# Three pairs of score banks, and row maxima as single-bank units, in a fused attention and mixture-of-experts kernel

## The chip, the cores and the metric

The kernel runs on one core of a Trainium2 chip. The time is device microseconds (us) of one execution, the median of several runs. The engines that matter here are TensorE (PE, with its weight loads as PEld), VectorE (DVE), ScalarE (ACT) and GpSimd (POOL); SyncE (SP) issues nearly all transfers. They run side by side and meet only at semaphores.

## The reference

The change lies in the first of three stages, attention over 32 heads (4 batches by 8), 1152 keys of 64 numbers, and 576 queries after pooling by two:

```python
q_pool = q.reshape(B, H, S // factor, factor, D).mean(axis=3)
scores = scale * np.matmul(q_pool, k.transpose(0, 1, 3, 2))
scores = scores - np.max(scores, axis=-1, keepdims=True)
attn = np.exp(scores)
attn = attn / (np.sum(attn, axis=-1, keepdims=True) + 1e-09)
return np.matmul(attn, v).astype(np.float32)
```

Two mixture-of-experts stages follow (from about 440 us on); the change doesn't touch them.

## The kernel before, in words

PSUM has eight banks of 512 fp32 per partition, and `ps` is all of them. The head size is 64, half of the array's 128 rows, so the operands lie twice: even and odd tiles of keys and of queries are on partitions 0 to 63 (half 0, `rows_of(0)`) and 64 to 127 (half 1, `rows_of(1)`). Matmuls of the two halves go to different banks.

**Scores.** A head n has nine steps, `scores(n, s)`. A step is eight matmuls, four parts (L652, L654, L656, L658: high by high, low by high, high by low, and the row maximum with its sign turned) on each half, each 288 columns wide, accumulated into a pair of banks, one bank for a half. ScalarE then takes the exponential of the pair into `probs` (`exp_step`, L1067). The pair alternates between banks 0/1 and 2/3 (`step_bank`), and a step waits until the exponential of the step two before it is done.

**Row maxima.** The maximum over the keys must be known before a head's scores are made, so it is found one head ahead: while head n's scores are made, `row_max(n + 1, j)` makes single-pass scores of head n+1, and VectorE reduces them (`top_of_rows`). There are six jobs to a head. Five are a matmul of 512 keys on each half (L620) into a pair of banks, reduced by one instruction of 2x512 (L1357); the one with j=4 is five small matmuls for the last 128 keys (L613, L615) and two reductions (L1351, L1353). The jobs alternate between bank pairs 6/7 and 4/5 and stand before the steps s = 0, 2, 3, 4, 6, 7 (`JOB_STEPS`). A job waits until the job two before it is reduced. `join_tops` (L1364) joins the maxima into `neg_max`.

**End of a head.** TensorE's queue then has `turn(n+2, 0)` and `turn(n+2, 1)` (transposes of the keys and queries of head n+2, L580 to L591, into banks 6 and 7 and a tail bank), `turn_neg_max(n+1)` (L629, a transpose that waits for `join_tops(n+1)`), `weigh(n)` (36 matmuls of the probabilities with the values into bank 4, L675) and `add_up(n)` (the sums, L686). ScalarE meanwhile rounds the turned operands (`round_k`, `round_q`), places the maxima (`place_neg_max`) and reads the result out of bank 4 (`read_x`). VectorE makes the low parts (`low_k`, `low_q`, `low_ends`) and adds one pair of probabilities (`add_pair`, L1384). GpSimd adds the other probabilities (L498 to L512) and divides.

Each engine's order is written out by hand: the loop at the end of the TensorE block, and the like for the others. TensorE works strictly in that order, so what stands behind a waiting instruction waits too.

Of the kernel before, what the change touches and what calls it, by code (L numbers as in the profile page):

```python
# [8 lines left out]
ALU = mybir.AluOpType  # L9
ACT = mybir.ActivationFunctionType  # L10
AX = mybir.AxisListType
P = 128
# [4 lines left out]
def soft_moe_chain(nc, q, k, v, phi, w1, w2, w_in, w_out, out):  # L17
# [47 lines left out]
    JOBS = QT + 1  # L65
    KP = (NT - 1) // 2 * P
# [102 lines left out]
    with ExitStack() as ctx:  # L169
# [39 lines left out]
        def job_bank(m, j):  # L209
            if m == 0:  # L210
                return 2 if j % 2 == 0 else 4
            return 6 if j % 2 == 0 else 4

        def step_bank(n, s):
            if n == HEADS - 1:
                return (2, 0, 6)[s % 3]
            return 2 * ((n + s) % 2)

        def tail_bank(m):
            if m < 2:  # L220
                return 1 - m
            return 2 * ((m + 1) % 2) + 1
# [4 lines left out]
        def turned_q(odd):  # L227
            return ps[rows_of(odd), 7, 0:QF // 2 * P].rearrange("r (a c) -> r a c", c=P)
# [339 lines left out]
        def _(pe):  # L568
            JOB_STEPS = (0, 2, 3, 4, 6, 7)

            def turn(m, j):

                if m == 1:
                    pe.wait_ge(max_free, 1)
                elif m > 1:
                    pe.wait_ge(max_free, JOBS * m - 1)
                if j == 0:
                    pe.wait_ge(k_loaded, 32 * m + 32)
                    for t in range(NT // 2):
                        mm = pe.transpose(ps[:, 6, P * t:P * t + P],  # L580
                                          k_raw[:, 2 * t:2 * t + 2, :].rearrange("p t d -> p (t d)"), ident[:])
                else:
                    pe.wait_ge(q_pooled, m + 1)
                    for t in range(QF // 2):
                        pe.transpose(ps[:, 7, P * t:P * t + P], q_pool[:, 2 * t:2 * t + 2, :].rearrange("p two d -> p (two d)"),  # L585
                                     ident[:])
                    if m >= 2:
                        pe.wait_ge(exp_done, NT * (m - 2) + NT - 1)
                    pe.transpose(ps[:, tail_bank(m), 0:P], k_raw[:, NT - 1:NT + 1, :].rearrange("p two d -> p (two d)"),
                                 ident[:])  # L590
                    mm = pe.transpose(ps[:, tail_bank(m), P:2 * P],  # L591
                                      q_pool[:, QF:QT + 1, :].rearrange("p two d -> p (two d)"), ident[:])
                mm.then_inc(turned, 1)

            def row_max(m, j):

                if m == 0 and j in (0, QF):
                    pe.wait_ge(rounded, 5 if j == 0 else ROUNDS)
                if j == 0:
                    if m > 0:  # L600
                        pe.wait_ge(turn_free, 2 * m + 2)
                elif j == 1:
                    if m > 1:
                        pe.wait_ge(x_read, m - 1)
                    if m > 0:
                        pe.wait_ge(max_free, JOBS * m)
                else:
                    pe.wait_ge(max_free, JOBS * m + (j - 1))
                if j == QF:
                    b = job_bank(m, j)  # L610
                    for t in (0, 2, 1, 3):
                        g = t // 2
                        pe.matmul(ps[:, b + g, P * (t % 2):P * (t % 2) + P], q_hi[m % 2][rows_of(g), P * t:P * t + P],  # L613
                                  k_hi[m % 2][rows_of(g), KP:KP + P], start=True, stop=True)
                    mm = pe.matmul(ps[:, b, 2 * P:3 * P], q_hi[m % 2][rows_of(0), P * QF:P * QT],  # L615
                                   k_hi[m % 2][rows_of(0), KP:KP + P], start=True, stop=True)
                else:
                    t = min(j, QF)
                    for g in range(2):
                        mm = pe.matmul(ps[:, job_bank(m, j) + g, :], q_hi[m % 2][rows_of(g), P * t:P * t + P],  # L620
                                       k_hi[m % 2][rows_of(g), 0:KP], start=True, stop=True)
# [9 lines left out]
            def scores(n, s):  # L631

                if s == 0:
                    pe.wait_ge(neg_free, n + 1)
                    if n > 0:
                        pe.wait_ge(turn_free, 2 * min(n + 2, HEADS))
                if n == 0 and s == 0:
                    pe.wait_ge(turn_free, 3)
                if n == HEADS - 1 and s >= 2:
                    pe.wait_ge(exp_done, NT * n + max(s - 2, 0))  # L640
                elif NT * n + s >= 2:
                    pe.wait_ge(exp_done, NT * n + s - 1)
                b0 = step_bank(n, s)
                for part in range(4):
                    for g in range(2):
# [15 lines left out]
            def weigh(n):  # L661
# [6 lines left out]
                if n + 1 < HEADS:  # L668
                    pe.wait_ge(max_free, JOBS * (n + 1) + JOBS)
# [59 lines left out]
            row_max(0, 0)  # L729
            row_max(0, 1)  # L730
            warm(5, 0)
            row_max(0, 2)
            turn(1, 0)
            row_max(0, 3)
            turn(1, 1)
            row_max(0, 4)
            row_max(0, 5)
# [313 lines left out]
        def _(act):  # L1051
# [31 lines left out]
            def round_k(m):  # L1083
                act.wait_ge(turned, 2 * m + 1)
                high(k_hi[m % 2][:, 0:KP], ps[:, 6, :])

            def round_q(m):
                kh, qh, b = k_hi[m % 2], q_hi[m % 2], tail_bank(m)
                act.wait_ge(turned, 2 * m + 2)
                for g in range(2):  # L1090
                    for odd in range(2):
                        high(by_turns(qh, g, odd), turned_q(odd))
                high(kh[:, KP:KP + P], ps[:, b, 0:P])
                high(qh[:, P * QF:SQ], ps[:, b, P:P + QLAST])
# [206 lines left out]
        def _(dve):  # L1301
# [29 lines left out]
            def low_k(m):  # L1331
                dve.wait_ge(rounded, ROUNDS * m + 1)
                low(k_lo[m % 2][:, 0:KP], ps[:, 6, :], k_hi[m % 2][:, 0:KP]).then_inc(turn_free, 1)

            def low_q(m):
                dve.wait_ge(rounded, ROUNDS * m + 5)
                for g in range(2):
                    for odd in range(2):
                        low(by_turns(q_lo[m % 2], g, odd), turned_q(odd), by_turns(q_hi[m % 2], g, odd))

            def low_ends(m):
                b = tail_bank(m)
                dve.wait_ge(rounded, ROUNDS * m + ROUNDS)
                low(k_lo[m % 2][:, KP:KP + P], ps[:, b, 0:P], k_hi[m % 2][:, KP:KP + P])
                low(q_lo[m % 2][:, P * QF:SQ], ps[:, b, P:P + QLAST], q_hi[m % 2][:, P * QF:SQ]).then_inc(turn_free, 1)

            def top_of_rows(m, j):
                dve.wait_ge(max_full, JOBS * m + j + 1)
                if j == QF:
                    b = job_bank(m, j)  # L1350
# [3 lines left out]
                else:  # L1354
                    t, b = min(j, QF), job_bank(m, j)
# [3 lines left out]

            def join_tops(m):  # L1360
                dve.wait_ge(max_free, JOBS * m + JOBS)
# [37 lines left out]

            def tops(m, invert):  # L1400
                for j in range(JOBS):
                    top_of_rows(m, j)
                    if j == 3 and invert:
# [5 lines left out]
            tops(0, False)  # L1409
# [224 lines left out]
```

## Time and profile before

| | |
|---|---|
| median of 3 runs (lowest to highest) | 740.65 us (740.49 to 741.43) |
| the profiled execution | 741.45 us, of which its span is 739.7 us |
| TensorE / VectorE / ScalarE / GpSimd busy over the span | 98% / 71% / 62% / 65% |
| heads | 32, one about every 13.5 us, to about 440 us |
| granted TensorE clock, mean | 0.993 |

Busy times are sums of instruction durations, and matmuls overlap: a TensorE that is shown busy may still stand between two streams. A matmul's duration includes its way through the array, so the pace is read from the distance between two starts, not from the durations. The chain of work that ended last follows, from the end backwards, what released each instruction. Times of day in the rows below are in microseconds from the start of the span.

### The profile page before, as it was taken

The numbers are of one execution on the slowest core, as the hardware profiler recorded it, in microseconds if no ns is written. First come the engines' busy times: TensorE is split into PE (matmuls) and PEld (weight loads), VectorE is DVE, ScalarE is ACT, GpSimd is POOL, SyncE is SP. The second block draws the span as 40 slices with busy tenths as digits, with TensorE's granted clock in tenths as the row PEclk, the third lists the DMA queues.
The fourth block names the chain that finished last, engine by engine and source line by source line (L and its number), as shares of the span: only waits on it lengthen the run. The fifth ranks groups of instructions, "written<-read, shape, count | busy, mean of one in ns | idle before, by whom it ended". The sixth has DMA issues, their size and how long they took to land.

```text
span 739.7 us, 17095 instructions
## 1 busy us (share of the span) xinstructions
PE 726.1 (98%) x6375; PEld 541.8 (73%) x6375; DVE 524.3 (71%) x828; ACT 455.1 (62%) x1008; POOL 483.7 (65%) x429
## 2 busy tenths in 40 slices
PE   6999999999999999999999999999999999999997
PEld 5777777777777767777777677434778888888886
DVE  7888888888888888888888847533895555455542
ACT  4677776776777767767767763214665454545453
POOL 1588888888888888888888872212774444444442
PEclk9899999999999999999999999999999999999999
DMA  5123435334334353343443347899301010101011
GB/s 147 41 59 84 122 92 156 103 106 155 88 104 159 90 156 104 98 164 88 124 139 88 96 140 263 299 386 375 138 0 43 1 43 0 43 0 43 0 43 43
DMA packets 51623, 81.83 MB, mean 111 GB/s; under 512 B 14556, under 2 KB 20572, under 8 KB 51548
## 3 DMA queue, kind: packets, MB, share of 16 engines
q1 hardware_dynamic: 51180, 80.37, 34.8%
q8 instruction: 48, 0.79, 0.4%
q10 hardware_dynamic: 368, 0.46, 0.2%
q14 instruction: 27, 0.22, 0.1%
HBM read 75.94 MB, written 4.79 MB: 109 GB/s over the span
## 4 chain that ended last, share of the span: by engine, by line
PE 94%; DVE 3%; issue 1%; POOL 1%; ACT 1%; POOLq 0%; DVEq 0%; ACTq 0%
PE ps L675 20%; PE ps L652 9%; PE ps L982 8%; PE ps L981 8%; PE ps L980 8%; PE ps L620 6%; PE ps L654 5%; PE ps L656 5%; PE ps L658 5%; PE ps L686 3%; PE ps L580 3%; PE ps L970 2%; PE ps L864 2%; PE ps L894 2%; PE ps L585 1%
## 5 line engine op out<-in xcount | busy, mean ns | idle before, releaser
L1067 ACT ACTIVATE probs<-ps 128x576 f32<-128x576 f32 x288 | 183.7, 651 | 45.1 <-PE ps L658 31.4
L1357 DVE TENSOR_REDUCE mx<-ps 128x2 f32<-128x1024 f32 (+1 forms) x160 | 189.4, 1218 | 29.9 <-PE ps L620 27.9
L546 POOL TENSOR_TENSOR g_lo<-g_buf,g_hi 128x384 fp32r<-128x384 f32 x96 | 102.1, 1065 | 100.9 <-ACT g_hi L1242 100.9
L675 PE MATMUL ps<-probs,v_sb 128*64 128x288 f32 x1152 | 146.8, 409 | 0.1
L509 POOL TENSOR_TENSOR p_sum<-p_sum,probs 128x576 f32<-128x576 f32 x93 | 129.1, 1415 | 0.0
L1585 DVE SCALAR_TENSOR_TENSOR v_buf<-u_buf 128x384 f32<-128x384 f32 x96 | 60.4, 629 | 86.4 <-ACT u_buf L1235 85.8
L675 PEld LDWEIGHTS ps<-probs,v_sb 128*64 128x64 f32 x1152 | 79.6, 137 | 56.4 <-issue 5.2
L1235 ACT ACTIVATE u_buf<-ps,half 128x384 f32<-128x384 f32 x96 | 55.7, 581 | 93.9 <-PE ps L970 93.9
L980 PE MATMUL ps<-wo_hi,g_hi 128*128 128x512 f32 x282 | 110.4, 391 | 0.6 <-POOL g_lo L546 0.5
L982 PE MATMUL ps<-wo_lo,g_hi 128*128 128x512 f32 x282 | 110.8, 393 | 0.0
L981 PE MATMUL ps<-wo_hi,g_lo 128*128 128x512 f32 x282 | 110.6, 392 | 0.0
L652 PE MATMUL ps<-q_hi,k_hi 64*128 64x288 f32 x576 | 102.0, 337 | 0.7 <-ACT q_neg L1100 0.7
L654 PE MATMUL ps<-q_hi,k_lo 64*128 64x288 f32 x576 | 88.6, 293 | 0.0
L656 PE MATMUL ps<-q_lo,k_hi 64*128 64x288 f32 x576 | 88.6, 293 | 0.0
L658 PE MATMUL ps<-q_neg,k_one 64*128 64x288 f32 x576 | 88.2, 291 | 0.0
L498 POOL TENSOR_TENSOR p_sum<-probs 128x576 f32<-128x576 f32 x32 | 45.6, 1425 | 50.3 <-ACT probs L1067 50.3
L620 PE MATMUL ps<-k_hi,q_hi 64*128 64x512 f32 x320 | 70.5, 427 | 3.2 <-DVE mx L1357 2.1
L652 PEld LDWEIGHTS ps<-q_hi,k_hi 64*128 64x128 f32 x576 | 56.0, 186 | 23.9 <-ACT probs L1067 21.7
L980 PEld LDWEIGHTS ps<-wo_hi,g_hi 128*128 128x128 f32 x282 | 53.0, 188 | 14.3 <-issue 2.7
L1329 DVE TENSOR_TENSOR q_lo<-ps,q_hi 64x256 fp32r<-64x256 f32 (+1 forms) x160 | 60.5, 379 | 2.5 <-ACT q_hi L1081 1.2
L982 PEld LDWEIGHTS ps<-wo_lo,g_hi 128*128 128x128 f32 x282 | 53.0, 188 | 11.4
L654 PEld LDWEIGHTS ps<-q_hi,k_lo 64*128 64x128 f32 x576 | 58.1, 187 | 2.7
(216 smaller groups left out, 1252.1 us busy)
## 6 DMA issues: line engine op xcount, KB each, us to landing
pre<-in_moe_w SPq DMA_DIRECT2D x41, 512.0 KB, 4.9
v_sb<-in_v SPq DMA_DIRECT2D x32, 288.0 KB, 2.9
k_raw<-in_k SPq DMA_DIRECT2D x31, 288.0 KB, 3.8
q_raw<-in_q SPq DMA_DIRECT2D x32, 256.0 KB, 4.0
from_x<-in_moe_w SPq DMA_DIRECT2D x9, 512.0 KB, 5.1
p_inv<-inv_dram SPq DMA_DIRECT2D x62, 72.0 KB, 2.7
out<-o_stage SPq DMA_DIRECT2D x34, 128.0 KB, 2.3
staged<-in_moe_w SPq DMA_DIRECT2D x8, 512.0 KB, 5.5
```

Source lines behind the costliest of these rows:

```text
L509: nc.gpsimd.tensor_tensor(total, total, probs[:, u, :], ALU.add).then_inc(probs_added, 1)
L620: mm = pe.matmul(ps[:, job_bank(m, j) + g, :], q_hi[m % 2][rows_of(g), P * t:P * t + P], k_hi[m % 2][rows_of(g), 0:KP], start=True, stop=True)
L652: mm = pe.matmul(out, k_hi[n % 2][rows, t], q_hi[n % 2][rows, cols], start=True, stop=False)
L654: mm = pe.matmul(out, k_lo[n % 2][rows, t], q_hi[n % 2][rows, cols], start=False, stop=False)
L656: mm = pe.matmul(out, k_hi[n % 2][rows, t], q_lo[n % 2][rows, cols], start=False, stop=False)
L658: mm = pe.matmul(out, k_one[rows, :], q_neg[n % 2][rows, cols], start=False, stop=True)
L675: mm = pe.matmul(ps[D * h:D * h + D, 4, 0:HALF], v_sb[n % 2][:, u, :], probs[:, u, HALF * h:HALF * h + HALF], start=(i == 0), stop=(i == N ...
L980: pe.matmul(o, g_hi[par][:, f, toks], wo_hi[:, f, :], start=(f == 0), stop=False)
L981: pe.matmul(o, g_lo[par][:, f, toks], wo_hi[:, f, :], start=False, stop=False)
L982: mm = pe.matmul(o, g_hi[par][:, f, toks], wo_lo[:, f, :], start=False, stop=(f == NF - 1))
L1067: nc.scalar.activation(dst, ps[:, b0:b0 + 2, 0:HALF], ACT.Exp, scale=SCORE_SCALE).then_inc(exp_done, 1)
L1357: top = nc.vector.tensor_reduce(mx[0:w, NC * t:NC * t + 2], ps[0:w, b:b + 2, :], AX.X, ALU.max)
```

## The change

- Scores use three pairs of banks in turn: 2(n mod 2), the other of 0/1 and 2/3, and 4/5. The wait of a step is now for the exponential of the step three before it. Steps 1 and 2 of a head wait for the turned operands of head n+2 to be split and for `read_x` instead.
- From head 1 on, the maxima are made in 12 single-bank units (`UNITS`) in place of 6 jobs in pairs: ten of one matmul of 512 keys on one half, then three and two small matmuls. Unit u uses half u mod 2 and bank 6 + u mod 2, and from u = 2 on waits until unit u-2 is reduced. Unit s stands before step s, and units 9, 10 and 11 stand behind the last step. Head 0 keeps the six jobs.
- VectorE reduces each unit by an instruction of its own, with one more for the last 64 queries: 13 for a head where there were 7.
- In heads 1 to 30, even steps begin with half 1.
- The turned operands and the maxima use the banks of the scores; the turns wait for exponentials, not for reductions.
- `weigh` no longer waits for the reductions, and `low_q` waits for all of ScalarE's roundings.

```diff
+    UNITS = 2 * QF + 4
...
-        def job_bank(m, j):
-            if m == 0:
-                return 2 if j % 2 == 0 else 4
-            return 6 if j % 2 == 0 else 4
+        def job_bank(j):
+            return 2 if j % 2 == 0 else 4
+
+        def unit_bank(u):
+            return 6 + u % 2
...
         def step_bank(n, s):
-            if n == HEADS - 1:
-                return (2, 0, 6)[s % 3]
-            return 2 * ((n + s) % 2)
-
-        def tail_bank(m):
+            if s % 3 == 2:
+                return 6 if n == HEADS - 1 else 4
+            return 2 * ((n + s % 3) % 2)
+
+        def keys_bank(m):
+            return 6 if m < 2 else 2 * (m % 2)
+
+        def queries_bank(m):
+            return 7 if m < 2 else 2 * (m % 2) + 1
...
-                if m == 1:
-                    pe.wait_ge(max_free, 1)
-                elif m > 1:
-                    pe.wait_ge(max_free, JOBS * m - 1)
+                if m >= 2:
+                    pe.wait_ge(exp_done, NT * (m - 2) + NT - 2)
...
+            def row_max(m, u):
+
+                if u == 0:
+                    pe.wait_ge(turn_free, 2 * m + 2)
+                if u >= 2:
+                    pe.wait_ge(max_free, units_of(m) + (u - 1))
+                b, g = unit_bank(u), u % 2
+                if u < UNITS - 2:
+                    t = u // 2
+                    mm = pe.matmul(ps[:, b, :], q_hi[m % 2][rows_of(g), P * t:P * t + P], k_hi[m % 2][rows_of(g), 0:KP],
+                                   start=True, stop=True)
+                else:
+                    tiles = (0, 1, QF) if g == 0 else (2, 3)
+                    for i, t in enumerate(tiles):
+                        mm = pe.matmul(ps[:, b, P * i:P * i + P], q_hi[m % 2][rows_of(g), P * t:P * t + P],
+                                       k_hi[m % 2][rows_of(g), KP:KP + P], start=True, stop=True)
                 mm.then_inc(max_full, 1)
...
-                if n == HEADS - 1 and s >= 2:
-                    pe.wait_ge(exp_done, NT * n + max(s - 2, 0))
-                elif NT * n + s >= 2:
-                    pe.wait_ge(exp_done, NT * n + s - 1)
+                    if n == 0:
+                        pe.wait_ge(turn_free, 3)
+                if s == 1 and 0 < n < HEADS - 1:
+                    pe.wait_ge(turn_free, 2 * n + 4)
+                if s == 2 and 0 < n < HEADS - 1:
+                    pe.wait_ge(x_read, n)
+                if s >= 3:
+                    pe.wait_ge(exp_done, NT * n + s - 2)
...
-                if n + 1 < HEADS:
-                    pe.wait_ge(max_free, JOBS * (n + 1) + JOBS)
...
                 for s in range(NT):
-                    if n + 1 < HEADS and s in JOB_STEPS and (n > 0 or s > 0):
-                        row_max(n + 1, JOB_STEPS.index(s))
-                    scores(n, s)
+                    if n + 1 < HEADS and (n > 0 or s > 0):
+                        row_max(n + 1, s)
+                    scores(n, s, (1, 0) if s % 2 == 0 and 0 < n < HEADS - 1 else (0, 1))
...
+                if n + 1 < HEADS:
+                    for u in range(NT, UNITS):
+                        row_max(n + 1, u)
                 if n + 2 < HEADS:
                     turn(n + 2, 0)
```

TensorE in the middle of head 1, before: a job's two matmuls (both halves), then a step, whose first matmul waits for an exponential.

```order
L620 MATMUL ps<-k_hi_62,q_hi_66 128x512 [waits max_free]
L620 MATMUL ps<-k_hi_62,q_hi_66 128x512
L652 MATMUL ps<-q_hi_67,k_hi_63 128x288 [waits exp_done]
L652 MATMUL ps<-q_hi_67,k_hi_63 128x288
L654 MATMUL ps<-q_hi_67,k_lo_65 128x288 x2
L656 MATMUL ps<-q_lo_71,k_hi_63 128x288 x2
L658 MATMUL ps<-q_neg_69,k_one 128x288 x2
```

The same place after the change (lines are those of the changed kernel): one matmul of one half stands before each step.

```order
L632 MATMUL ps<-k_hi_62,q_hi_66 128x512 [waits max_free]
L669 MATMUL ps<-q_hi_67,k_hi_63 128x288 [waits exp_done]
L669 MATMUL ps<-q_hi_67,k_hi_63 128x288
L671 MATMUL ps<-q_hi_67,k_lo_65 128x288 x2
L673 MATMUL ps<-q_lo_71,k_hi_63 128x288 x2
L675 MATMUL ps<-q_neg_69,k_one 128x288 x2
L632 MATMUL ps<-k_hi_62,q_hi_66 128x512 [waits max_free]
```

The matmul of 512 was a pair before five of the nine steps, and is now a single one before each of them.

TensorE at the end of head 1, before: the last step is followed by the turns at once.

```order
L658 MATMUL ps<-q_neg_69,k_one 128x288 x2
L580 MATMUL ps<-ident,k_raw 128x128 [waits k_loaded,max_free]
L580 MATMUL ps<-ident,k_raw 128x128 x3
L585 MATMUL ps<-ident,q_pool 128x128 [waits q_pooled,max_free]
L585 MATMUL ps<-ident,q_pool 128x128
L589 MATMUL ps<-ident,k_raw 128x128 [waits exp_done]
L591 MATMUL ps<-ident,q_pool 128x128
```

After the change:

```order
L675 MATMUL ps<-q_neg_69,k_one 128x288 x2
L632 MATMUL ps<-k_hi_62,q_hi_66 128x512 [waits max_free]
L637 MATMUL ps<-k_hi_62,q_hi_66 128x128 [waits max_free]
L637 MATMUL ps<-k_hi_62,q_hi_66 128x128 x2
L637 MATMUL ps<-k_hi_62,q_hi_66 128x128 [waits max_free]
L637 MATMUL ps<-k_hi_62,q_hi_66 128x128
L589 MATMUL ps<-ident,k_raw 128x128 [waits k_loaded,exp_done]
L589 MATMUL ps<-ident,k_raw 128x128 x3
L596 MATMUL ps<-ident,q_pool 128x128 [waits q_pooled,exp_done]
```

Units 9, 10 and 11 now stand between the last step and the turns, each with a wait for VectorE.

VectorE's maxima of one head, before, and then after:

```order
L1357 TENSOR_REDUCE mx<-ps 128x2 [waits max_full] x4
L1370 RECIPROCAL p_spread<-p_spread 64x9 [waits sums_spread]
L1351 TENSOR_REDUCE mx<-ps 128x4 [waits max_full]
L1353 TENSOR_REDUCE mx<-ps 64x1
L1357 TENSOR_REDUCE mx<-ps 64x2 [waits max_full]
L1364 TENSOR_REDUCE neg_max<-mx 128x2x5 [waits neg_full,max_free]
```

```order
L1383 TENSOR_REDUCE mx<-ps 128x1 [waits max_full] x8
L1403 RECIPROCAL p_spread<-p_spread 64x9 [waits sums_spread]
L1383 TENSOR_REDUCE mx<-ps 64x1 [waits max_full] x2
L1385 TENSOR_REDUCE mx<-ps 128x2 [waits max_full]
L1389 TENSOR_REDUCE mx<-ps 64x1
L1385 TENSOR_REDUCE mx<-ps 128x2 [waits max_full]
L1397 TENSOR_REDUCE neg_max<-mx 128x2x5 [waits neg_full,max_free]
```

Seven reductions and the joining one became thirteen and the joining one; the reciprocal of the sums keeps its place after two thirds of the wide ones.

## Rows read from the trace of the kernel before

**Rows 1.** The page: chain of waits, shares of the span by engine and line

```profile
PE 94%; DVE 3%; issue 1%; POOL 1%; ACT 1%; POOLq 0%; DVEq 0%; ACTq 0%
```

**Rows 2.** One head in four stretches: busy us (instructions) of PE, PEld, DVE, ACT, POOL; clock

```profile
209.62:216.82 7.20, 7.20 (x92) 6.21 (x88) 6.59 (x8) 5.79 (x10) 5.56 (x6) 1.00 0.19 47
216.82:217.95 1.13, 1.13 (x12) 0.96 (x10) 0.30 (x2) 1.02 (x2) 1.13 (x2) 1.00 0.01 0
217.95:222.46 4.51, 4.51 (x37) 2.49 (x36) 3.98 (x7) 3.21 (x12) 4.26 (x4) 1.00 0.38 120
222.46:223.09 0.63, 0.63 (x18) 0.40 (x16) 0.31 (x2) 0.00 (x0) 0.55 (x2) 1.00 0.98 387
```

**Rows 3.** Timeline of TensorE in that head: start, us (of the group), line, operands, count

```profile
209.62 0.50 PE L620 MATMUL ps<-k_hi,q_hi 64*128 64x512 f32 x2
209.96 0.30 PE L652 MATMUL ps<-q_hi,k_hi 64*128 64x288 f32 x2
...
210.49 0.30 PE L652 MATMUL ps<-q_hi,k_hi 64*128 64x288 f32 x2
...
211.01 0.40 PE L620 MATMUL ps<-k_hi,q_hi 64*128 64x512 f32 x2
211.40 0.40 PE L652 MATMUL ps<-q_hi,k_hi 64*128 64x288 f32 x2
...
214.50 0.27 PE L615 MATMUL ps<-k_hi,q_hi 64*128 64x128 f32 x1
214.52 0.43 PE L652 MATMUL ps<-q_hi,k_hi 64*128 64x288 f32 x2
...
215.15 0.43 PE L620 MATMUL ps<-k_hi,q_hi 64*128 64x512 f32 x2
215.38 0.33 PE L652 MATMUL ps<-q_hi,k_hi 64*128 64x288 f32 x2
```

**Rows 4.** Timeline of the weight loads, same head, with idle time before and its releaser

```profile
211.40 0.19 PEld L652 LDWEIGHTS ps<-q_hi,k_hi 64*128 64x128 f32 x2 [0.32 <-ACT probs L1067]
211.51 0.19 PEld L654 LDWEIGHTS ps<-q_hi,k_lo 64*128 64x128 f32 x2
...
216.81 0.42 PEld L580 LDWEIGHTS ps<-ident,k_raw 128*128 128x128 f32 x4 [0.16 <-issue]
...
217.64 0.14 PEld L629 LDWEIGHTS ps<-ident,neg_max 128*128 128x128 f32 x1
217.95 0.20 PEld L675 LDWEIGHTS ps<-probs,v_sb 128*64 128x64 f32 x4 [0.17 <-issue]
```

**Rows 5.** Waits from 20 to 440 us: total us, times, longest

```profile
PEld ps L652 <- ACT probs L1067: 21.7, 92, 0.3
```

**Rows 6.** Timeline of ScalarE: two exponentials

```profile
210.69 1.20 ACT L1067 ACTIVATE probs<-ps 128x576 f32<-128x576 f32 x2 [0.17 <-PE ps L658]
```

**Rows 7.** Timeline of VectorE, same head

```profile
212.60 2.35 DVE L1357 TENSOR_REDUCE mx<-ps 128x2 f32<-128x1024 f32 x2
...
214.86 0.20 DVE L1370 RECIPROCAL p_spread<-p_spread 64x9 f32<-64x9 f32 x1
214.98 0.62 DVE L1351 TENSOR_REDUCE mx<-ps 128x4 f32<-128x512 f32 x1
215.52 0.28 DVE L1353 TENSOR_REDUCE mx<-ps 64x1 f32<-64x128 f32 x1
215.72 1.21 DVE L1357 TENSOR_REDUCE mx<-ps 64x2 f32<-64x1024 f32 x1
216.97 0.19 DVE L1364 TENSOR_REDUCE neg_max<-mx 128x10 f32<-128x30 f32 x1
218.14 0.69 DVE L1329 TENSOR_TENSOR k_lo<-ps,k_hi 128x512 fp32r<-128x512 f32 x1 [0.99 <-ACT k_hi L1081]
```

**Rows 8.** Timeline of GpSimd: its last sum of the head

```profile
220.15 1.80 POOL L512 TENSOR_TENSOR p_sum<-p_sum,p_sum 128x576 f32<-128x576 f32 x1
```

More of the change, by code:

```diff
@@ L583, in turn @@
                     pe.wait_ge(q_pooled, m + 1)
+                    if m == 1:
+                        pe.wait_ge(max_free, 1)
                     for t in range(QF // 2):
[L585 to L590, printed above, removed]
@@ L593, in turn, with row_max_first @@
                 mm.then_inc(turned, 1)
-            def row_max(m, j):
-                if m == 0 and j in (0, QF):
+            def row_max_first(j):
+                if j in (0, QF):
                     pe.wait_ge(rounded, 5 if j == 0 else ROUNDS)
[L599 to L608, printed above, removed]
+                if j > 1:
+                    pe.wait_ge(max_free, j - 1)
+                b = job_bank(j)
@@ L609, in row_max @@
                 if j == QF:
-                    b = job_bank(m, j)
                     for t in (0, 2, 1, 3):
                         g = t // 2
[L613 to L616, printed above, removed]
+                        pe.matmul(ps[:, b + g, P * (t % 2):P * (t % 2) + P], q_hi[0][rows_of(g), P * t:P * t + P],
+                                  k_hi[0][rows_of(g), KP:KP + P], start=True, stop=True)
@@ L617, in row_max @@
+                    mm = pe.matmul(ps[:, b, 2 * P:3 * P], q_hi[0][rows_of(0), P * QF:P * QT],
+                                   k_hi[0][rows_of(0), KP:KP + P], start=True, stop=True)
                 else:
@@ L629, in turn_neg_max, with scores @@
                 pe.transpose(ps[:, neg_bank(m), 0:P], neg_max[:, :], ident[:]).then_inc(neg_full, 1)
-            def scores(n, s):
+            def scores(n, s, halves):
                 if s == 0:
                     pe.wait_ge(neg_free, n + 1)
[L635 to L638, printed above, removed]
-                if n == HEADS - 1 and s >= 2:
-                    pe.wait_ge(exp_done, NT * n + max(s - 2, 0))
-                elif NT * n + s >= 2:
-                    pe.wait_ge(exp_done, NT * n + s - 1)
+                    if n == 0:
[6 more added lines that the diff above has]
+                    pe.wait_ge(exp_done, NT * n + s - 2)
                 b0 = step_bank(n, s)
                 for part in range(4):
-                    for g in range(2):
+                    for g in halves:
                         rows = rows_of(g)
@@ L1354, in top_of_rows @@
                 else:
-                    t, b = min(j, QF), job_bank(m, j)
+                    t = min(j, QF)
                     w = q_cols(t)[1]
@@ L1398, in top_logits, with tops_first @@
                                         negate=True).then_inc(l_neg_ready, 1)
+            def tops_first():
+                for j in range(JOBS):
+                    top_of_rows_first(j)
+                join_tops(0)
             def tops(m, invert):
-                for j in range(JOBS):
-                    top_of_rows(m, j)
-                    if j == 3 and invert:
+                for u in range(UNITS):
+                    top_of_rows(m, u)
+                    if u == 7 and invert:
                         invert_sums(m - 2)
@@ L1408, in _ @@
             low_q(0)
-            tops(0, False)
+            tops_first()
             low_ends(0)
```

83 lines of the change are left out of this document (52 added, 31 removed).

## The prediction

> **What bounds the kernel now.** I read the chain of waits first: 94% of it is TensorE [rows 1], so its queue is the path, and what counts is where it stands still within a head. The windows of one head [rows 2] give the share of each stretch: 7.20 us from the first job to the last step, 1.13 us for the turns and the transposed maxima, 4.51 us for weighing, 0.63 us for the sums, 13.47 us together. The clock is granted in full in all four (1.00), so no term below needs another level. I write all times of a head as distances from its first weight load, at 209.62.
>
> The timeline gives TensorE's pace by distances of starts [rows 3]. A step without a wait takes 0.53 us (209.96 to 210.49), so one of its four parts takes 0.13 on both halves together. A job of 512 holds its halves for 0.23 (215.15 to 215.38). Nine steps and six jobs are 9 x 0.53 + 5 x 0.23 + about 0.2 = 6.1 us, and the stretch is 7.20: **1.1 us is waiting**. The rows show which: the load of L652 at 211.40 stood idle 0.32 us for an exponential [rows 4], and over the 31 heads there were 92 such waits, three a head, 21.7 us of idle weight loads in all [rows 5]; the weights that such a wait keeps from being loaded ahead, and VectorE in front of some jobs, make up the rest. With two pairs a pair's round is matmul, exponential, next matmul, and TensorE meets it.
>
> **What the change takes away.** Two exponentials whose scores are there start 0.55 apart (1.20 less 0.65) [rows 6], less than any step takes. With a third pair a step waits for the exponential three steps back: that one ends about 0.4 (last part of a step) + 0.3 + 0.65 + 0.1 = 1.45 us after its scores began, and three steps take at least 1.6. So the waits for exponentials go, and I take the steps to run at the pace of the streams.
>
> **What a unit costs beside a step.** A single unit loads one half only. The trace has a lone matmul of this kind: L615, on half 0 at 214.50, and the next step's first matmul starts on half 1 0.02 us later [rows 3]; from there the halves run apart by some 0.04. So a unit and the other half's part run together, and the alternation of halves in the new order lets the lead change sides. Over two steps each half carries one unit and eight parts: 0.23 + 8 x 0.1325 = 1.29, or **0.645 us a step**. The first step of a head is 0.63 by the same reckoning (unit 0 truly starts at 0.11, since its weights were not loaded ahead: the step between two loads behind a wait is 0.11 [rows 4]). Unit 9 then starts at 0.11 + 0.63 + 8 x 0.645 = 5.90. The whole stretch of steps, 7.20 before, is 1.3 us shorter. This is the gain.
>
> **What VectorE makes of it.** A reduction of 1024 follows the one before after 1.13 (2.35 less 1.22), one of 128 holds the next back 0.20 (215.52 to 215.72) [rows 7]. That is 1.04 ns per element, and 0.60 for a unit of 512; its duration is 0.62, as for the 512 elements of L1351. Ten units, the reciprocal (0.12) and the three small ones (0.33 + 0.20 + 0.33) are 7.0 us, in place of 5 x 1.13 + 0.54 + 0.20 + 0.12 = 6.5. At 0.60 a unit it keeps pace with TensorE's 0.645, and starts each unit 0.43 after TensorE (0.39 of matmul, 0.04 of signal). Two single banks suffice: from a unit's weight load to the freeing of its bank are 0.11 + 0.39 + 0.04 + 0.62 + 0.05 = 1.21, and TensorE comes back to it after 1.29.
>
> **The end of the head is where it is paid back.** Units 9, 10 and 11 have no step beside them, and two banks between them. VectorE: unit 7 starts at 4.61 + 0.43 = 5.04, the reciprocal at 5.64, unit 8 at 5.76, unit 9 at 6.36, which ends at 6.98. TensorE: unit 9 at 5.90, unit 10 at 6.43 behind the reduction of unit 8, and the load for unit 11 only at 7.03, behind that of unit 9. Its second matmul is loaded at 7.14. The first turn changes the shape of the array, and that costs: from the load of L629 to that of L675 0.31 pass, with 0.17 idle that nothing releases [rows 4]; I take 0.26, as the small matmul streams no longer than L629's but is in a half of its own. So the turns are loaded from 7.40 on, and L629's load comes 0.83 later (216.81 to 217.64 [rows 4]), at **8.23**. Before it came at 217.64 less 209.62 = **8.02**.
>
> VectorE's own end is just in front of that: unit 10 is ready at 6.76 + 0.27 and takes 0.33 + 0.20, unit 11 starts at 7.56 and ends at 7.92, the join (0.19) is out at 8.18 with its signal. The two paths are 0.05 apart, so either may end last.
>
> Behind L629 nothing changes: weighing needs the last exponential, ready about 7.0 now, and the sums need GpSimd, whose last sum ends at 221.95 with the sums' load at 222.46 [rows 2, 8]; it now starts earlier. VectorE's chain from the split of the keys to the freeing of the turned operands hangs on weighing, as before. Of 31 heads with units each loses 0.21 us: 6.5 us. Head 0 doesn't change its halves, and a unit on the half that goes first is then in front of the step instead of beside it: 0.1 at four steps, under 0.5 in all. Against it stands a small gain: heads in which the sums waited for GpSimd a little.
>
> The profiled execution took 741.45 us, 0.8 above the median of 740.65. The sum is 741.45 + 6.5 = 748, and against the median **747 us**.
>
> **Where it may be wrong by size.** The price I didn't see is a one-bank reduction in a stream. Its lower bound is 0.55, the distance behind L1351 (214.98 to 215.52), where no semaphore stands between; since TensorE sets the pace, that changes the end of unit 9 by 0.02 to 0.05. Its upper bound is the 0.69 us of the 512-wide subtraction from PSUM [rows 7]; at 0.66 to 0.69 VectorE is slower than TensorE, unit 9 is reduced from 6.6 on, and L629 comes about 0.4 later than before: +12.5 us, 753. I take 0.60, as it lies on the line of the reductions themselves. The Trainium skill ("VectorE: DVE Perf Modes", section on the TRN2 errata) gives an instruction that reads PSUM 120 cycles beside its elements, at 0.96 GHz. By that one unit would be 0.66 us, an estimate from the page, and the sum would end at 753. The trace disagrees in the 1024-wide case, where the page's formula gives 1.19 and the pace is 1.13; so the page's case is left to the rival that follows from the 0.69.
>
> **The rivals.**
> 1. *VectorE sets the pace* (0.66 or more a unit): 753 us, as just worked out. For it: the subtraction's row. Against it: the line through the reductions.
> 2. *Faster.* The place is the same, units 9 to 11. If TensorE's units come earlier than I think, because a lone unit runs wholly beside the step, VectorE alone sets the end: unit 9 starts at 0.54 + 9 x 0.60 + 0.12 = 6.06, unit 11 is loaded at 6.73, and L629 at 7.93, 0.09 before its time now: 31 x 0.09 = 2.8 us, 738. It decides at a step's pace below 0.60. Against it: each half must carry 1.29 us of streams in two steps. That unit 9 needn't be waited for at all, and the whole 1.1 us is won (706 us), would need reductions that no row shows.
> 3. *No overlap of halves*: a unit alone holds both. A step is then 0.53 + 0.23 = 0.76, unit 9 starts at 6.95 and its reduction ends at 8.0, L629 at 9.25: +1.2 us a head, 778 us. L615 speaks against it.
> 4. *Ping-pong.* The margin of two single banks is 0.08 us a round (1.21 against 1.29). If TensorE nonetheless meets VectorE at most units, each meeting costs the weight load of 0.11 that isn't hidden: 0.75 a step, +1 us a head, 770 us.
> 5. *No change*: the 0.21 is the difference of two sums of some 8 us, and 0.05 less twice leaves little over 3 us.
>
> **The numbers.** A measurement of this kernel can tell about 0.2% (1.5 us) from no change. The forecast case, 743 to 750 us, has 0.50; rival 1 0.12; rival 2 0.17; rivals 3 and 4 0.06 each; no change 0.09. That is 0.17 faster, 0.09 the same, 0.74 slower. The range takes in rivals 1, 2 and 5 with their bounds, 737 to 757; it leaves out rivals 3 and 4 and the far end of 2.
>
> **What would show it.** Right: steps 0.64 apart and hardly any idle of L669's loads behind ScalarE; about 0.3 and 0.35 us of waiting in front of units 10 and 11 behind VectorE's reductions; exponentials 0.64 apart that end near 7.0; weighing 8.5 to 8.6 after the head's start; one head every 13.67 us. Wrong: reductions of one bank 0.66 apart and TensorE waiting at most units (rivals 1, 4), steps of 0.76 (rival 3), or a wait of the transposed maxima for the join with the turns long done, which would mean that VectorE's tail is longer than I have it. If the third pair didn't free TensorE, exponentials would still stand in its waits.

## The result

| | median, us | lowest to highest |
|---|---|---|
| before, measured beside it (4 runs) | 741.04 | 740.49 to 741.58 |
| the change (4 runs) | 748.36 | 747.04 to 749.08 |

The ratio is 1.0097 (95% interval 1.0078 to 1.0115): the change makes the kernel 1% slower. The prediction was 747 us, in a range of 737 to 757. The profiled executions are 741.45 and 747.77 us, 6.3 apart; the sum gave 6.5.

The chain of waits on the page of the changed kernel, by engine and then by line:

```profile
PE 67%; DVE 29%; issue 1%; POOL 1%; ACT 1%; DMA 1%; ACTq 0%; DVEq 0%; POOLq 0%
DVE mx L1383 26%; PE ps L690 20%; PE ps L1000 8%; PE ps L999 8%; PE ps L998 8%; PE ps L701 3%; PE ps L589 3%; PE ps L988 2%; PE ps L912 2%; PE ps L882 2%; PE ps L632 2%; PE ps L637 2%; PE ps L596 1%; PE ps L791 1%; DVE v_buf L1623 1%
```

TensorE had 94% of the chain [rows 1]. Now a quarter of the whole span leads back through the maxima's reductions on VectorE (L1383). That share is not what a faster reduction would bring (e1 below): the ten wide reductions of a head follow each other without a gap, so a chain that enters at the last one is led back through all of them (26% of 746 us is 6.3 us for each of 31 heads). A head in stretches, from the first unit to the next head's: steps; units 9 to 11; turns and maxima; weighing; sums. Columns as in [rows 2].

```profile
211.89:217.76 5.87, 5.87 (x84) 5.87 (x82) 5.32 (x10) 5.28 (x10) 4.11 (x6) 1.00 0.23 62
217.76:219.29 1.53, 1.31 (x11) 0.79 (x8) 1.49 (x4) 0.97 (x2) 1.53 (x3) 1.00 0.03 2
219.29:220.42 1.13, 1.13 (x10) 0.98 (x10) 0.75 (x4) 0.44 (x1) 1.13 (x1) 1.00 0.08 14
220.42:224.94 4.52, 4.52 (x38) 2.50 (x37) 4.00 (x8) 3.21 (x12) 4.19 (x5) 1.00 0.55 184
224.94:225.56 0.62, 0.62 (x18) 0.40 (x16) 0.00 (x0) 0.00 (x0) 0.62 (x1) 1.00 1.06 300
```

The steps take 5.87 us where they took 7.20: the gain is there, 1.33 us. The units behind them take 1.53, and the other three stretches are what they were (1.13, 4.52, 0.62). The sum is 0.20 us a head more. It is the same in every head: from one weighing to the next there are 13.47 to 13.50 us before and 13.67 to 13.69 after, in 29 heads in a row, 5.7 us in all. The next distance is 0.6 us longer as well, the last head with all that follows takes 0.3 us more, and what stands before the first weighing 0.25 less, which makes the 6.3. The weight loads at the head's end, with idle time and what ended it:

```profile
217.65 0.18 PEld L632 LDWEIGHTS ps<-k_hi,q_hi 64*128 64x128 f32 x1
...
218.32 0.41 PEld L637 LDWEIGHTS ps<-k_hi,q_hi 64*128 64x128 f32 x3 [0.47 <-DVE mx L1383]
218.92 0.29 PEld L637 LDWEIGHTS ps<-k_hi,q_hi 64*128 64x128 f32 x2 [0.19 <-DVE mx L1383]
219.29 0.42 PEld L589 LDWEIGHTS ps<-ident,k_raw 128*128 128x128 f32 x4
...
220.13 0.14 PEld L646 LDWEIGHTS ps<-ident,neg_max 128*128 128x128 f32 x1
220.42 4.08 PEld L690 LDWEIGHTS ps<-probs,v_sb 128*64 128x64 f32 x36 [0.15 <-issue]
```

The loads for units 10 and 11 are 6.43 and 7.03 us after the head's start (211.89), the first turn's 7.40, the transposed maxima's 8.24. These four are the times of the prediction to 0.01 us. VectorE's timeline and ScalarE's, same head:

```profile
212.43 5.16 DVE L1383 TENSOR_REDUCE mx<-ps 128x1 f32<-128x512 f32 x8 [1.44 <-PE ps L632]
217.51 0.20 DVE L1403 RECIPROCAL p_spread<-p_spread 64x9 f32<-64x9 f32 x1
217.63 1.24 DVE L1383 TENSOR_REDUCE mx<-ps 64x1 f32<-64x512 f32 x2
218.91 0.43 DVE L1385 TENSOR_REDUCE mx<-ps 128x2 f32<-128x256 f32 x1
...
219.89 0.19 DVE L1397 TENSOR_REDUCE neg_max<-mx 128x10 f32<-128x30 f32 x1
```

```profile
212.96 5.82 ACT L1085 ACTIVATE probs<-ps 128x576 f32<-128x576 f32 x9 [0.16 <-PE ps L675]
```

Nine exponentials fill 5.82 us without a pause of note, 0.65 apart on average, and end 6.9 us after the head's start. The reductions and the join go on to 8.2.

### The profile page after: what moved, and what is told of

Read it like the earlier page. It is cut to its first block, busy times and chain, and to the rows that moved or that the text cites. A ratio compares the mean times of both kernels' runs of the same rounds, so it can differ in the third digit from the quotient of the medians.

```text
span 746.0 us, 17190 instructions
## 1 busy us (share of the span) xinstructions
PE 725.1 (97%) x6375; PEld 555.6 (74%) x6375; DVE 528.6 (71%) x1014; ACT 451.4 (61%) x1008; POOL 482.0 (65%) x429
## 4 chain that ended last, share of the span: by engine, by line
PE 67%; DVE 29%; issue 1%; POOL 1%; ACT 1%; DMA 1%; ACTq 0%; DVEq 0%; POOLq 0%
DVE mx L1383 26%; PE ps L690 20%; PE ps L1000 8%; PE ps L999 8%; PE ps L998 8%; PE ps L701 3%; PE ps L589 3%; PE ps L988 2%; PE ps L912 2%; PE ps L882 2%; PE ps L632 2%; PE ps L637 2%; PE ps L596 1%; PE ps L791 1%; DVE v_buf L1623 1%
## 5 line engine op out<-in xcount | busy, mean ns | idle before, releaser
L1383 DVE TENSOR_REDUCE mx<-ps 128x1 f32<-128x512 f32 x310 | 198.5, 682 | 44.1 <-PE ps L632 43.6
L632 PE MATMUL ps<-k_hi,q_hi 64*128 64x512 f32 x310 | 126.0, 408 | 0.3 <-DVE mx L1383 0.3
L669 PE MATMUL ps<-q_hi,k_hi 64*128 64x288 f32 x576 | 123.6, 298 | 0.7 <-ACT q_neg L1118 0.7
L671 PE MATMUL ps<-q_hi,k_lo 64*128 64x288 f32 x576 | 120.2, 292 | 0.0
L673 PE MATMUL ps<-q_lo,k_hi 64*128 64x288 f32 x576 | 120.1, 292 | 0.0
L675 PE MATMUL ps<-q_neg,k_one 64*128 64x288 f32 x576 | 119.4, 291 | 0.0
L673 PEld LDWEIGHTS ps<-q_lo,k_hi 64*128 64x128 f32 x576 | 86.6, 184 | 0.0
L675 PEld LDWEIGHTS ps<-q_neg,k_one 64*128 64x128 f32 x576 | 86.4, 184 | 0.0
L671 PEld LDWEIGHTS ps<-q_hi,k_lo 64*128 64x128 f32 x576 | 86.4, 184 | 0.0
L669 PEld LDWEIGHTS ps<-q_hi,k_hi 64*128 64x128 f32 x576 | 74.1, 185 | 1.7 <-issue 1.7
```

Source lines behind the costliest of these rows:

```text
L632: mm = pe.matmul(ps[:, b, :], q_hi[m % 2][rows_of(g), P * t:P * t + P], k_hi[m % 2][rows_of(g), 0:KP], start=True, stop=True)
L669: mm = pe.matmul(out, k_hi[n % 2][rows, t], q_hi[n % 2][rows, cols], start=True, stop=False)
L671: mm = pe.matmul(out, k_lo[n % 2][rows, t], q_hi[n % 2][rows, cols], start=False, stop=False)
L673: mm = pe.matmul(out, k_hi[n % 2][rows, t], q_lo[n % 2][rows, cols], start=False, stop=False)
L675: mm = pe.matmul(out, k_one[rows, :], q_neg[n % 2][rows, cols], start=False, stop=True)
L1383: top = nc.vector.tensor_reduce(mx[0:w, NC * t + g:NC * t + g + 1], ps[0:w, b, :], AX.X, ALU.max)
```

## The experiments

All ratios are to the kernel before, run beside each kernel. Edits are to the changed kernel where nothing else is said. A head's time is counted from its first weight load.

**e1: shorter reductions.** The maxima leave out half the keys.

```diff
-top = nc.vector.tensor_reduce(mx[0:w, NC * t + g:NC * t + g + 1], ps[0:w, b, :], AX.X, ALU.max)
+top = nc.vector.tensor_reduce(mx[0:w, NC * t + g:NC * t + g + 1], ps[0:w, b, 0:2 * P], AX.X, ALU.max)
```

> The changed kernel, but VectorE reduces only 256 of the 512 columns of each wide unit, so that half the keys are left out of the maxima; TensorE's work is the same. Theory (the end of the head pays the gain back, as units 9 to 11 wait for reductions): each reduction is some 0.27 us shorter, the waits in front of units 10 and 11 shrink to 0.2 us together, and the transposed maxima are loaded about 7.95 us after the head's start in place of 8.24: 9 us less than the changed kernel, 739 us. The steps stay 0.64 us apart. Rival (VectorE's pace holds up all steps): the steps come closer together too, and the gain is over 20 us. Rival (the loss is TensorE's own: lone units and the turns' new place): no gain, 748 us.

737.1 us, ratio 0.9933 (0.9919 to 0.9947), 11 us less than the change. Weight loads at the end of a head whose first load is at 208.58:

```profile
214.25 0.18 PEld L632 LDWEIGHTS ps<-k_hi,q_hi 64*128 64x128 f32 x1
214.74 0.41 PEld L637 LDWEIGHTS ps<-k_hi,q_hi 64*128 64x128 f32 x3 [0.21 <-DVE mx L1383]
215.30 0.29 PEld L637 LDWEIGHTS ps<-k_hi,q_hi 64*128 64x128 f32 x2 [0.15 <-DVE mx L1383]
...
216.55 0.14 PEld L646 LDWEIGHTS ps<-ident,neg_max 128*128 128x128 f32 x1
```

The maxima are loaded at 7.97, and the steps keep their pace: the last part of the last step (L675) is loaded at 5.77 in the median head, in the changed kernel at 5.78. So the gain, 0.31 us a head (13.37 in place of 13.68), comes from behind the steps. VectorE's pace doesn't hold the steps, but its reductions hold units 10 and 11, and a little unit 9 (loaded at 5.67, in the changed kernel at 5.76). The two rows that show this for unit 9 are, in the changed kernel, the reduction of unit 7, which ends at 217.59, and the load of unit 9 into the same bank:

```profile
216.91 0.68 DVE L1383 TENSOR_REDUCE mx<-ps 128x1 f32<-128x512 f32 x1
217.65 0.18 PEld L632 LDWEIGHTS ps<-k_hi,q_hi 64*128 64x128 f32 x1
```

It is the same for units 2 to 9 of every head: all 248 such loads come 0.05 us behind the end of the reduction of two units before. In e1 the median is 0.30. So TensorE meets VectorE at every unit of the changed kernel. The list of waits doesn't show it, since other weights are still being loaded meanwhile, and in the steps it costs nothing, since the other half's parts run on; only unit 9, which has no such parts after it, is 0.07 us later for it (5.87 against 5.80).

**e2: exponentials two back.**

```diff
-                    pe.wait_ge(exp_done, NT * n + s - 2)
+                    pe.wait_ge(exp_done, NT * n + s - 1)
```

> The changed kernel, with steps 3 to 8 of a head waiting for the exponential two steps back again, as with two pairs of banks. Theory (the third pair frees TensorE from ScalarE): the waits for exponentials come back, a step is 0.7 to 0.8 us, unit 9 starts near 6.9 us in place of 5.9, and a head is 0.9 to 1.0 us longer: 775 to 780 us. Rival (the third pair brings little, since the 1.1 us of waiting before lay with the jobs): under 10 us more than the changed kernel.

778.1 us, ratio 1.0487 (1.0471 to 1.0502). Weight loads in the steps of a head that began at 212.05, and then, on TensorE, its unit 9:

```profile
214.36 0.18 PEld L669 LDWEIGHTS ps<-q_hi,k_hi 64*128 64x128 f32 x2 [0.22 <-ACT probs L1085]
...
214.87 0.18 PEld L632 LDWEIGHTS ps<-k_hi,q_hi 64*128 64x128 f32 x1
215.11 0.18 PEld L669 LDWEIGHTS ps<-q_hi,k_hi 64*128 64x128 f32 x2
```

```profile
218.84 0.39 PE L632 MATMUL ps<-k_hi,q_hi 64*128 64x512 f32 x1
```

Unit 9 starts at 6.79 in place of 5.87. So the third pair is worth 0.92 us (6.79 less 5.87) a head here, some 29 us over 31 heads, and 29.8 is what the two medians differ by. The waits for the exponentials are back, now two steps back: from step 3 on a step's loads come 0.24 to 0.29 us behind its unit's (214.87 to 215.11), in the changed kernel 0.05 to 0.11, and the steps are 0.77 apart. The list of waits has only one such idle a head (30, 6.8 us in all), since in the later steps the unit's own load, of 0.18 us, covers most of it.

**e3: half 0 always first.**

```diff
-                    scores(n, s, (1, 0) if s % 2 == 0 and 0 < n < HEADS - 1 else (0, 1))
+                    scores(n, s, (0, 1))
```

> The changed kernel, with every step beginning with half 0, also behind a unit on half 0. Theory (a lone unit runs beside the other half's part only where that part is issued first): every second step waits for its unit's stream, 0.1 us more at four or five steps of a head, unit 9 starts 0.4 us later, and a head is 0.4 to 0.5 us longer: 12 to 16 us more than the changed kernel, 760 to 764 us. Rival (the halves sort themselves out, each carries the same streams in either order): the time of the changed kernel within 2 us. Rival (halves don't overlap with lone units at all): no difference either, and steps 0.76 us apart in both.

749.5 us, ratio 1.0101 (1.0087 to 1.0116): the change's time. The theory fell, its first rival holds. TensorE at the start of a head:

```profile
213.11 0.50 PE L632 MATMUL ps<-k_hi,q_hi 64*128 64x512 f32 x1
213.12 0.40 PE L669 MATMUL ps<-q_hi,k_hi 64*128 64x288 f32 x1
213.36 0.29 PE L671 MATMUL ps<-q_hi,k_lo 64*128 64x288 f32 x1
213.45 0.29 PE L669 MATMUL ps<-q_hi,k_hi 64*128 64x288 f32 x1
...
213.62 0.29 PE L675 MATMUL ps<-q_neg,k_one 64*128 64x288 f32 x1
213.71 0.29 PE L673 MATMUL ps<-q_lo,k_hi 64*128 64x288 f32 x1
213.76 0.38 PE L632 MATMUL ps<-k_hi,q_hi 64*128 64x512 f32 x1
213.85 0.29 PE L675 MATMUL ps<-q_neg,k_one 64*128 64x288 f32 x1
```

Both matmuls of L669 stand in the program in front of both of L671, half 0 before half 1. The trace doesn't name the halves, but the unit is the head's first and so runs on half 0, from 213.11. A matmul of L669 starts at 213.12, one of L671 at 213.36, and only then, at 213.45, the second of L669. So it must be the one on half 1 that went past the one on half 0, while the halves each keep their own order. The order of halves in the program is without effect on the time. Unit 9 is loaded at 5.75 in the median head of both kernels, which also rules out the second rival, steps of 0.76.

**e4: units 10 and 11 in the bank pair of step 7.**

```diff
-                if u >= 2:
+                if u >= UNITS - 2:
+                    pe.wait_ge(exp_done, NT * (m - 1) + NT - 1)
+                elif u >= 2:
                     pe.wait_ge(max_free, units_of(m) + (u - 1))
...
-            return 6 + u % 2
+            return 6 + u % 2 if u < UNITS - 2 else 2 * (m % 2) + u % 2
```

> The changed kernel, with units 10 and 11 in the bank pair of step 7 in place of banks 6 and 7, so that they wait for that step's exponential and not for the reductions of units 8 and 9. Theory (the waits at the end pay the gain back): unit 11 is loaded near 6.6 us in place of 7.03, the turns near 6.9 in place of 7.40, and then the join of the maxima is what the transposed maxima wait for, near 8.05 in place of 8.24: 0.2 us a head less, 742 us, no better than the kernel before. TensorE stands 0.4 us a head in front of the transposed maxima. Rival (VectorE's tail is no bound): the transposed maxima at 7.7, 731 us. Rival (something behind them holds the head, ScalarE or GpSimd): 748 us.

742.7 us, ratio 1.0015 (1.0003 to 1.0027), 5.6 less than the change and a little slower than before. Weight loads of the end of a head that began at 211.54:

```profile
217.78 0.41 PEld L639 LDWEIGHTS ps<-k_hi,q_hi 64*128 64x128 f32 x5 [0.27 <-ACT probs L1087]
218.26 0.42 PEld L589 LDWEIGHTS ps<-ident,k_raw 128*128 128x128 f32 x4
...
219.67 0.14 PEld L648 LDWEIGHTS ps<-ident,neg_max 128*128 128x128 f32 x1 [0.56 <-DVE neg_max L1399]
219.93 2.14 PEld L692 LDWEIGHTS ps<-probs,v_sb 128*64 128x64 f32 x20
```

The turns are loaded at 6.72 in place of 7.40 (6.9 was expected). The maxima then wait 0.56 us for the join, and are loaded at 8.13 (8.05 was expected): the second path, 0.05 us behind the first in the prediction, has become the bound.

**e5 and e6: the maxima inside the weighing.** Both on top of e4. e5 moves `turn_neg_max(n + 1)` behind the second of the weighing's nine tiles; e6 also makes it of two matmuls with the weighing's shape. The edit is e6's; e5 has `turn_neg_max(n + 1)` in the second line.

```diff
                     mm.then_inc(pv_done, 1)
+                    if i == 1 and n + 1 < HEADS:
+                        turn_neg_max_narrow(n + 1)
...
+                for h in range(2):
+                    mm = pe.matmul(ps[rows_of(h), neg_bank(m), 0:P], neg_max[:, D * h:D * h + D], ident[:], start=True, stop=True)
+                mm.then_inc(neg_full, 1)
...
-                if n + 1 < HEADS:
-                    turn_neg_max(n + 1)
                 weigh(n)
```

> e4, and the transposed maxima moved from in front of the weighing to behind its second tile, so that weighing no longer stands behind the join. Theory: TensorE had the turns loaded by 7.43 us after the head's start and weighing begins at 7.75 in place of 8.39, but the transpose has another array shape than its neighbours, and the two switches inside the weighing cost 0.3 us each: of the 0.64 us some 0.1 to 0.2 us a head are left, 737 to 740 us. Rival (the switch costs nothing where the queue is full): 0.5 us a head, 727 us. Rival (ScalarE needs the maxima earlier): no gain.

> As e5, but the maxima are turned by two matmuls of 64 columns against the identity, the array shape of the weighing. Theory: no switch, so weighing begins at 7.75 and lasts 0.15 us longer, 0.5 us a head less than e4 on TensorE. GpSimd then is next: from its first sum (3.06 us after the head's start) to the end of its divisions it takes 10.65 us, and ScalarE waits for those before it reads the result and makes the next exponentials; that round is 13.2 us a head in place of 13.53: 732 us (728 to 736). Rival (GpSimd doesn't matter): 13.03 a head, 727 us. Rival (TensorE isn't held by the join): as e4, 742 us.

e5: 734.2 us, ratio 0.9905 (0.989 to 0.992). e6: **728.5 us**, ratio 0.983 (0.9817 to 0.9844), faster than both kernels. The loads around the maxima, of e5 and then of e6:

```profile
226.97 0.68 PEld L692 LDWEIGHTS ps<-probs,v_sb 128*64 128x64 f32 x8 [0.17 <-issue]
228.09 0.14 PEld L648 LDWEIGHTS ps<-ident,neg_max 128*128 128x128 f32 x1 [0.44 <-issue]
228.35 3.11 PEld L692 LDWEIGHTS ps<-probs,v_sb 128*64 128x64 f32 x28
```

```profile
224.24 0.68 PEld L700 LDWEIGHTS ps<-probs,v_sb 128*64 128x64 f32 x8 [0.17 <-issue]
225.02 0.39 PEld L655 LDWEIGHTS ps<-ident,neg_max 128*64 128x64 f32 x4
225.38 3.16 PEld L700 LDWEIGHTS ps<-probs,v_sb 128*64 128x64 f32 x28
```

From the first weighing load to the ninth are 1.38 us in e5 and 1.14 in e6: the other shape has 0.44 us of idle in front of it, and the like one shows none. From its first load to that of the sums weighing takes 4.67 us in the changed kernel, 5.08 in e5 and 4.88 in e6 (median heads). The weighing begins 7.74 us after the head's start in e6 (224.24 less 216.50), as expected. Both expectations missed in a term. The maxima with their two switches cost e5 0.41 us of weighing where 0.6 was expected for the switches alone, and its time is 2.8 us under the range given. In e6 a head takes 13.10, so the round through GpSimd that was to hold it at 13.2 did not hold it. The time lies in the range, but a head is the rival's 13.03 with 0.21 us of longer weighing in place of 0.15.

**e7 and e8: the narrow maxima alone**, in the changed kernel and in the kernel before.

> The changed kernel with the narrow maxima inside the weighing, units 10 and 11 left in banks 6 and 7. Theory (here TensorE's own chain, reduction of unit 9 to unit 11 to the turns, ends last, and the join is only just in front of it): nothing is won, weighing begins at 8.45 in place of 8.53 and lasts 0.15 us longer, 748 to 751 us. Rival (the join holds the changed kernel): 735 us or less.

> The kernel before the change, with the narrow maxima inside the weighing. Theory: there the join was not waited for, and nothing is won: weighing begins 0.1 us earlier and lasts 0.15 us longer, 741 to 743 us. Rival (moving the maxima is a gain by itself, whatever the banks): under 736 us.

e7: 748.8 us, ratio 1.0101 (1.0085 to 1.0116). e8: 745.4 us, ratio 1.0048 (1.0033 to 1.0063), 2.4 us more than I gave it at most. In e8 weighing begins 0.10 earlier, as expected, but takes 4.88 us there too, 0.21 more than in the kernel before where I had 0.15, and a head is 0.12 longer. In e7 a head is likewise 0.11 longer than in the changed kernel (13.79), though the medians are only 0.4 us apart. So the maxima's new place is worth nothing without e4's banks, and by itself loses a little in either kernel.

**e9: e6 with exponentials two back** (the edit of e2).

> e6 with steps 3 to 8 waiting for the exponential two steps back, as in e2. Theory: with the end of the head out of the way the third pair is worth its full time, since the steps are now the path alone: unit 9 starts 1 us later in every head and 28 to 32 us are lost, 757 to 761 us. Rival (in e6 the third pair no longer matters, the gain is the maxima's new place): under 5 us lost.

751.1 us, ratio 1.0131 (1.0111 to 1.0151): 22.6 us lost, less than the 28 I gave as the least, and four times what the rival allows. In e6 units 10 and 11 wait 0.27 us a head for the exponential of step 7. With slower steps that wait is gone, and this accounts for the miss: unit 9 is loaded 0.90 us later (6.66 for 5.76), but unit 10 only 0.70 (6.93 for 6.23), and a head is 0.70 longer.

**e10 and e11: the reciprocal of the sums behind the join**, in the changed kernel and in e6.

```diff
                     top_of_rows(m, u)
-                    if u == 7 and invert:
-                        invert_sums(m - 2)
                 join_tops(m)
+                if invert:
+                    invert_sums(m - 2)
```

> The changed kernel, with VectorE's reciprocal of the sums (0.12 us) behind the join of the maxima in place of in front of unit 8. Theory (the reductions of units 8 and 9 are on the path): unit 11 is loaded 0.05 us earlier, since behind that TensorE's own unit 9 sets the reduction, and a head is 0.05 us shorter: 1.5 us, 746.5 to 747.5. Rival (the reductions are off the path): no difference. Rival (the transfers that hang on the reciprocal come back too late for GpSimd's divisions): slower than the changed kernel, GpSimd waiting for p_inv in most heads, 750 us or more.

> e6 with the reciprocal behind the join. Theory: units 10 and 11 wait for an exponential and the join is hidden behind weighing, so VectorE's tail is off the path and nothing is won: 728 to 729 us. Rival (VectorE still sets the end): 727 us or less. Rival (p_inv comes back too late): 731 us or more, with GpSimd's waits for it at over 0.3 us a head.

756.9 us (ratio 1.0207, 1.0193 to 1.0221) and 751.6 us (1.014, 1.012 to 1.0161). Both theories fell, and the rival with the transfers holds. Waits from 20 to 440 us in total, times and longest: e10's two rows, then e11's. The five executions of e11 lie between 751.3 and 756.1 us, and its rows are from the longest.

```profile
PEld ps L701 <- POOL p_sum L523: 14.2, 16, 1.8
POOL x_t L491 <- DMA p_inv<-inv_dram: 33.8, 26, 3.1
```

```profile
PEld ps L713 <- POOL p_sum L523: 30.8, 22, 3.3
POOL x_t L491 <- DMA p_inv<-inv_dram: 30.5, 21, 4.1
```

SyncE sends the inverted sums to memory and back. From the end of the reciprocal to the landing of the last copy that takes 4.8 to 6.8 us in e10, 5.2 in the median, and the reciprocal itself comes 2.5 us later in the head than in the changed kernel. So GpSimd's divisions wait for the copies, then its sums are late and TensorE waits for those.

The delay doesn't reach TensorE in every head of e10, and the others answer the question that was asked: 19 of 29 take the 13.67 to 13.69 us of the changed kernel, with unit 11 loaded at 7.04 as there. Where the reciprocal no longer stands in front of unit 8, its reduction starts 0.03 us earlier, but that of unit 9 follows a one-bank reduction only after 0.61 us, and comes 6.31 us after the head's start as before. The reciprocal in front of unit 8 costs the changed kernel nothing.

**e12: e6 with the reciprocal behind unit 5.**

> e6 with the reciprocal two units earlier, behind unit 5. Theory from the runs before (the reciprocal starts a round of transfers whose slack in front of GpSimd's divisions is small, and in e6 GpSimd waited for them 4 times, 2.1 us in all): at most those 2 us are won, 726.5 to 728.5 us. Rival (the round is slack in e6): 728.5 us as e6. Rival (the spread sums have not landed by then, and VectorE waits for them in the middle of the units): slower, over 730 us, with VectorE's reciprocal waiting for a transfer in most heads.

728.5 us, ratio 0.9828 (0.9813 to 0.9843), the time of e6. GpSimd's waits for the inverses, 2.1 us in four waits in e6, are gone, and nothing is won. With the reciprocal behind unit 7, where eight of the ten wide reductions are done, the round of transfers has just enough slack.

## Why the prediction was right

Step by step, in its own order:

- *Waits for exponentials go*: right. In the changed kernel no weight load of L669 shows a wait for them, and e2 brings them back, at 30 us.
- *0.645 us a step, unit 9 at 5.90*: measured 5.87. The reason was half right. A lone unit does run beside the other half's parts. That the alternation of halves in the new order is what allows it was wrong; by e3 each half runs in its own order, whatever the program's.
- *Two single banks suffice, 1.21 us for a round where TensorE comes back after 1.29*: wrong in size, and lucky. From the load of unit 7 (216.35) to that of unit 9 (217.65), 0.05 behind the reduction that frees its bank, are 1.30 us. The margin of 0.08 isn't there, and TensorE meets VectorE at every unit, which is what rival 4 starts from. That it costs nothing in the steps was not in the working; e1, where the banks are free earlier, has the same steps.
- *A reduction of 0.62 us, the next after 0.60*: the pace was right, the duration too short. L1383 lasts 0.68 on average, and one that stands waiting starts 0.61 after the one before it (1.29 for the first two of a head, less 0.68). Unit 9's starts 0.57 after unit 8's (1.24 for the two, less 0.67), at 6.31 in place of 6.36, and lasts 0.67. So it ends at 6.98, as forecast: two errors of 0.05 us cancelled, which is luck. The page of the Trainium skill that was cited ("VectorE: DVE Perf Modes", section on the TRN2 errata) gives 0.66 for the instruction, an estimate from its figures. The trace agrees with it roughly as a duration, not as the pace: rival 1, which took it as the pace, did not come true.
- *Units 10 and 11 behind the reductions, the turns at 7.40, the maxima at 8.23*: measured 6.43, 7.03, 7.40, 8.24. The two waits share out otherwise than forecast, 0.47 and 0.19 us in front of the loads where about 0.3 and 0.35 were given, with the same sum. e1 shortens the reductions and 11 us go; e4 takes these two waits away and 5.6 us go, till the join stops it at 8.13. Both paths stood where they were put.
- *Nothing changes behind the maxima*: right in sum. GpSimd was to gain a little. Its waits for the returned inverses grew instead, from 0.4 us in one wait to 4.7 in seven, without reaching TensorE. The heads are equally long all the same. This round was not in the working, and e10 shows that it had little slack.
- *6.5 us*: 6.3 between the profiled executions, 7.3 between the medians.

The rivals: 2 (faster) would have needed steps under 0.60 on average, and e1, with short reductions, is still at 0.64. Rivals 3 and 4 would show steps of 0.75 or more; of rival 4 the condition holds and the price doesn't, as told above. Rival 1's own terms come to a little more than its 753: with 0.66 a unit the maxima are loaded 0.45 us later than before, which is 14 us.

## What to carry to other kernels

When an engine stands still in many small waits, price what takes their place at the end of the stage as well: here 1.33 us a head came free in the steps and 1.53 had to be spent behind them, since the last units had nothing beside them and two banks between them. A buffer that is free for another reason (here a bank pair whose exponential is done) and work of the same array shape put in front of the late operand turned the same change from 1% slower into 1.7% faster. And before a small instruction is moved off a busy engine, follow what it starts: the reciprocal takes 0.12 us and begins a round of transfers that, when it came late, cost 9 us in the changed kernel and 23 in e6. A list of waits that is empty doesn't show slack either: here every unit was loaded at the moment its bank came free, and the list showed nothing of it.

## What the runs showed that was not expected

- Matmuls on different row halves start out of program order, so TensorE doesn't work as strictly in order as the description of the kernel has it. In e3 a part on half 1 starts 0.33 us before the one on half 0 that stands in front of it (213.12 and 213.45). The signal still keeps the order: of the last parts of that step one starts at 213.62 and the one before it in the program at 213.85, lasting 0.29, and the exponential that waits for the last starts only at 214.18, 0.045 us behind the end of the later one. In 131 of the 236 steps of e3 from 60 to 420 us the part with the signal is the first to start, and each time the exponential starts 0.045 us behind the end of the other:

```profile
214.18 0.65 ACT L1085 ACTIVATE probs<-ps 128x576 f32<-128x576 f32 x1 [0.17 <-PE ps L675]
```

- A reduction of one bank of 512 lasts 0.68 us, where one of the same number of elements in four pieces lasted 0.62 [rows 7], yet its pace is that of the line through the wider ones (0.61 against 0.60).
- An identity matmul in fp32 with 64 columns shows two weight loads (four for the two halves in e6, L655), as each of the weighing's own does (36 loads for 18 in the program), while the transpose it replaces shows one. The narrow form isn't free: weighing takes 0.21 us longer with it.
